# Padding v to pairs of chunks: one outer product and one near product where there were two

## What is computed

```python
state = 0
for t in range(S):
    cur = u * k[t] outer v[t]
    y[t] = r[t] @ (state + cur)
    state = w[t][:, None] * state + k[t] outer v[t]
x = y, heads side by side: (B*S, H*D)
x = moe(x)                       # 8 experts, 4 slots each
out = relu(x @ w_in) ** 2 @ w_out
```

## Time and profile before

| what | value |
|---|---|
| median of three runs | 556.15 us (553.27 to 556.74) |
| the profiled execution | 555.19 us, of it 553.4 us from the first to the last instruction |
| PE, busy | 485.5 us (88%) |
| ACT, busy | 332.8 us (60%) |
| DVE, busy | 334.6 us (60%) |
| the recurrence | to about 264 us; the rest is the two layers behind it |

### The profile page before, as it was taken

One profiled execution on the slowest core, in us unless ns is written; L12 is line 12 of the kernel. 1 busy time (PEld: TensorE's weight loads), 2 busy tenths in 40 slices (PEclk: granted clock), 3 DMA queues, 4 the chain that ended last, 5 costly groups with the idle time before them and its releaser, 6 DMA issues.

```text
span 553.4 us, 18757 instructions
## 1 busy us (share of the span) xinstructions
PE 485.5 (88%) x7850; PEld 425.1 (77%) x7850; DVE 334.6 (60%) x583; ACT 332.8 (60%) x689; POOL 13.7 (2%) x21
## 2 busy tenths in 40 slices
PE   1778889798989898678698879999999999999996
PEld 0557768677777777667333469999999999999996
DVE  5688868587878788925341167555555555555552
ACT  1787677686868687434221276656565656565653
POOL 9000000000000000000000000000000000000000
PEclk9998989798989899959889979999999999999999
DMA  6885565736262621293799730101010101010101
GB/s 112 146 213 103 150 113 152 137 70 117 57 118 52 114 56 34 59 403 136 238 390 369 260 114 1 44 1 44 1 43 2 43 0 43 0 43 1 44 1 43
DMA packets 119788, 56.23 MB, mean 102 GB/s; under 512 B 102944, under 2 KB 116256, under 8 KB 119328
## 3 DMA queue, kind: packets, MB, share of 16 engines
q1 hardware_dynamic: 116512, 42.54, 31.1%
q10 hardware_dynamic: 3200, 12.58, 6.1%
HBM read 50.38 MB, written 4.72 MB: 100 GB/s over the span
## 4 chain that ended last, share of the span: by engine, by line
PE 72%; ACT 11%; issue 7%; SPq 4%; DVE 4%; DMA 0%; ACTq 0%; DVEq 0%
PE bank L707 12%; PE bank L708 12%; PE bank L709 12%; ACT wide L802 4%; PE ybank L485 4%; PE lbank L468 4%; PE ybank L501 4%; PE lbank L451 4%; PE bank L697 4%; SPq L289 4%; PE tbank L402 3%; PE tbank L415 2%; PE bank L646 2%; PE bank L623 2%; ACT wl L743 2%
## 5 line engine op out<-in xcount | busy, mean ns | idle before, releaser
L707 PE MATMUL bank<-wo_high,h_high 128*128 128x384 f32 x384 | 129.6, 337 | 1.8 <-DVE h_low L1207 1.6
L708 PE MATMUL bank<-wo_low,h_high 128*128 128x384 f32 x384 | 129.0, 336 | 0.0
L709 PE MATMUL bank<-wo_high,h_low 128*128 128x384 f32 x384 | 128.9, 336 | 0.0
L953 ACT ACTIVATE h_relu<-bank 128x384 f32<-128x384 f32 x128 | 62.9, 492 | 74.4 <-PE bank L697 74.1
L1205 DVE CAST h_high<-h_sq 128x384 fp32r<-128x384 f32 x128 | 46.0, 359 | 96.7 <-PE bank L709 88.0
L1041 DVE TENSOR_TENSOR rk<-rk,wl 112x768 f32<-112x768 f32 x80 | 76.3, 954 | 36.7 <-PE lbank L468 19.9
L707 PEld LDWEIGHTS bank<-wo_high,h_high 128*128 128x128 f32 x384 | 72.6, 189 | 3.2 <-issue 2.7
L1207 DVE TENSOR_TENSOR h_low<-h_sq,h_high 128x384 fp32r<-128x384 f32 x128 | 71.5, 558 | 4.5
L708 PEld LDWEIGHTS bank<-wo_low,h_high 128*128 128x128 f32 x384 | 72.7, 189 | 0.0
L709 PEld LDWEIGHTS bank<-wo_high,h_low 128*128 128x128 f32 x384 | 72.5, 189 | 0.0
L957 ACT ACTIVATE h_sq<-h_relu 128x384 f32<-128x384 f32 x128 | 67.4, 527 | 4.1
(11 more groups left out here) (123 smaller groups left out, 532.5 us busy)
## 6 DMA issues: line engine op xcount, KB each, us to landing
w_sb<-in_moe_w_dram ACTq DMA_DIRECT2D x8, 1536.0 KB, 8.7
w_hi<-in_moe_w_dram SPq DMA_DIRECT2D x16, 384.0 KB, 8.0
nat<-in_w_dram SPq DMA_DIRECT2D x64, 72.0 KB, 2.4
nat<-in_r_dram SPq DMA_DIRECT2D x64, 72.0 KB, 2.5
nat<-in_k_dram SPq DMA_DIRECT2D x64, 72.0 KB, 2.4
v_tok<-in_v_dram SPq DMA_DIRECT2D x32, 144.0 KB, 3.1
w_lo<-in_moe_w_dram SPq DMA_DIRECT2D x1, 4608.0 KB, 16.8
out_dram<-o_sb SPq DMA_DIRECT2D x8, 576.0 KB, 3.0
```

The lines of the kernel that those rows point to most:

```text
L707: nc.tensor.matmul(acc, hi, wo_high[:, fb, :], start=(fb == 0), stop=False)
L708: nc.tensor.matmul(acc, hi, wo_low[:, fb, :], start=False, stop=False)
L709: last = nc.tensor.matmul(acc, lo, wo_high[:, fb, :], start=False, stop=(fb == NF - 1))
L953: nc.scalar.activation(h_relu[fb % 2][:], h_bank[fb % 2][:, 0:GT * P], ACT.Relu).then_inc(relu_done, 1)
```

## The change

v is kept with a padding: `v_tok` has for each block and head 96 columns. Tokens of the first chunk (partitions 0 to 63) hold v in columns 0 to 47 and zeros behind it, tokens of the second chunk (64 to 127) zeros and then v in columns 48 to 95. So one product with K = 128 rows and 96 columns gives both chunks' results side by side.

- `k_times_v`: 12 products of 48 x 96 in place of 22 of 48 x 48. Chunk c stands at column 48 (c mod 6) of bank c // 6, and `kv_out` copies it from there.
- `y_near`: 12 products of 64 x 96 in place of 24 of 64 x 48. Head h is now in PSUM partitions 64h to 64h+63, and the two chunks of a block side by side.
- `y_far`: the same 24 products with the same operands, but to PSUM partitions of the head instead of the chunk. The rows and the columns of the array that a product uses are now both those of head h.
- `y_to_x`: four copies of 64 partitions, one for each head and chunk, in place of two of 128.
- `load_v`: two transfers of 64 partitions per head in place of one of 128. Those of the first round move behind the inputs of the second round, and wait for GpSimd's zeros.
- GpSimd fills three more tiles (`v_tok`), and sets `ones` after the recurrence instead of as its second instruction.

```diff
-        v_tok = [[sb(f"v_tok{s}{b}", [P, PER, 2, D], c=att) for b in range(1 + s)] for s in range(2)]
+        v_tok = [[sb(f"v_tok{s}{b}", [P, PER, 2, 2, D], c=att) for b in range(1 + s)] for s in range(2)]
...
             def load_v(rd, s, h):
-                sp.dma_start(v_tok[s][rd % (1 + s)][:, :, h, :], v_v[rd * 4 + 2 * s + h]).then_inc(v_loaded[s], 16)
+                for par in range(2):
+                    sp.dma_start(v_tok[s][rd % (1 + s)][C * par:C * par + C, :, h, par, :], v_v[rd * 4 + 2 * s + h, par])\
+                        .then_inc(v_loaded[s], 16)
...
-            for s in range(2):
-                for h in range(2):
-                    load_v(0, s, h)
             sp.dma_start(phi_sb[:], phi.rearrange("(q p) n -> p q n", p=P)).then_inc(phi_loaded, 16)
...
+            sp.wait_ge(rows_zero, 13)
+            for s in range(2):
+                for h in range(2):
+                    load_v(0, s, h)
             for h in range(2):
                 load_v(1, 1, h)
...
-            pool.memset(ones[:], 1.0).then_inc(pool_const, 1)
...
-            for n, tile in enumerate(rt + rk0 + rk1 + rk2 + wide):
+            for n, tile in enumerate(rt + rk0 + rk1 + rk2 + wide + [v_tok[0][0], v_tok[1][0], v_tok[1][1]]):
                 if n:
                     pool.wait_ge(rows_zero, n)
                 pool.memset(tile[96:P] if n < 8 else tile[:], 0.0).then_inc(rows_zero, 1)
+            after_attention(pool)
+            pool.wait_ge(rows_zero, 13)
+            pool.memset(ones[:], 1.0).then_inc(ones_set, 1)
...
-                for c in range(NC - 1):
-                    i, par = divmod(c, 2)
-                    rows = slice(C * par, C * par + C)
+                for i in range(PER):
                     for h, (a, b) in enumerate(HEADS):
-                        last = nc.tensor.matmul(ybank[a:b, 512 * par + i * D:512 * par + (i + 1) * D],
-                                                k_tok[s][rows, i, a:b], v_tok[s][rd % (1 + s)][rows, i, h, :], start=True, stop=True)
+                        at = 512 * (i // GT) + (i % GT) * PW
+                        last = nc.tensor.matmul(ybank[a:b, at:at + PW], k_tok[s][:, i, a:b],
+                                                v_tok[s][rd % (1 + s)][:, i, h].rearrange("p par d -> p (par d)"),
+                                                start=True, stop=True)
...
                 for i in range(PER):
                     for h in range(2):
-                        for par in range(2):
-                            rows = slice(C * par, C * par + C)
-                            at = 512 * h + i * D
-                            last = nc.tensor.matmul(ybank[rows, at:at + D], aa[rd % 2][s][rows, PER * h + i, :],
-                                                    v_tok[s][rd % (1 + s)][rows, i, h, :], start=(i == 0), stop=False,
-                                                    skip_group_check=True)
+                        at = 512 * (i // GT) + (i % GT) * PW
+                        last = nc.tensor.matmul(ybank[HB * h:HB * h + C, at:at + PW], aa[rd % 2][s][:, PER * h + i, :],
+                                                v_tok[s][rd % (1 + s)][:, i, h].rearrange("p par d -> p (par d)"),
+                                                start=(i % GT == 0), stop=False, skip_group_check=True)
...
                             c = 2 * i + par
-                            rows = slice(C * par, C * par + C)
-                            at = 512 * h + i * D
-                            last = nc.tensor.matmul(ybank[rows, at:at + D], rk[rd % 3][s][a:b, 0, C * c:C * c + C],
-                                                    kv[s][a:b, :, c], start=False, stop=(i == PER - 1),
+                            at = 512 * (i // GT) + (i % GT) * PW + par * D
+                            last = nc.tensor.matmul(ybank[HB * h:HB * h + C, at:at + D], rk[rd % 3][s][a:b, 0, C * c:C * c + C],
+                                                    kv[s][a:b, :, c], start=False, stop=(i % GT == GT - 1),
                                                     skip_group_check=True)
...
-                for par, n in enumerate((NC // 2, NC // 2 - 1)):
-                    src = ybank[0:112, 512 * par:512 * par + n * D].rearrange("p (i d) -> p d i", d=D)
-                    dst = kv[s][0:112, :, 1 + par:2 + par + 2 * (n - 1):2]
-                    nc.scalar.activation(dst, src, ACT.Copy).then_inc(kv_evac[s], 1)
+                for half, n in enumerate((NC // 2, NC // 2 - 1)):
+                    src = ybank[0:112, 512 * half:512 * half + n * D].rearrange("p (c d) -> p d c", d=D)
+                    at = 1 + half * NC // 2
+                    nc.scalar.activation(kv[s][0:112, :, at:at + n], src, ACT.Copy).then_inc(kv_evac[s], 1)
...
                 for h in range(2):
-                    src = ybank[:, 512 * h:512 * h + PER * D].rearrange("p (i n) -> p i n", n=D)
-                    at = s * PW + h * D
-                    nc.scalar.activation(X[:, :, rd, at:at + D], src, ACT.Copy).then_inc(y_evac[s], 1)
+                    for par in range(2):
+                        src = ybank[HB * h:HB * h + C].rearrange("p (half x) -> p half x", half=2)[:, :, 0:GT * PW]\
+                            .rearrange("p half (i n) -> p half i n", n=PW)[:, :, :, par * D:par * D + D]
+                        at = s * PW + h * D
+                        dst = X[C * par:C * par + C, :, rd, at:at + D].rearrange("p (half i) n -> p half i n", half=2)
+                        nc.scalar.activation(dst, src, ACT.Copy).then_inc(y_evac[s], 1)
```

More of the change, by code:

```diff
@@ L39, in fused_kernel @@
     r_v, k_v, w_v = (a.rearrange("b h (g p i) d -> (b h) p g i d", p=P, i=2) for a in (r, k, w))
-    v_v = v.rearrange("b h (i p) d -> (b h) p i d", p=P)
+    v_v = v.rearrange("b h (i par p) d -> (b h) par p i d", par=2, p=C)
     T_ORDER = ([(s, 2, half) for s in range(2) for half in range(2)]
@@ L92, in fused_kernel @@
         u_col = sb("u_col", [P, 2 * ROUNDS])
-        ones = sb("ones", [P, P])
         comb = sb("comb", [P, SL])
@@ L160, in fused_kernel @@
         spread = sb("spread", [P, 2, 4, SL], F32R)
+        ones = sb("ones", [P, P])
         mx, mrow, mb = small[:, 0:1], small[0:1, 8:40], small[:, 40:72]
@@ L180, in fused_kernel @@
         rows_zero = sem("rows_zero")
+        ones_set = sem("ones_set")
         u_turned = sem("u_turned")
@@ L249, in after_attention @@
             for s in range(2):
-                eng.wait_ge(y_evac[s], 2 * ROUNDS)
+                eng.wait_ge(y_evac[s], 4 * ROUNDS)
         def xt_view(n):
@@ L329, in _ @@
                 for s in range(2):
-                    sp.wait_ge(y_evac[s], 2 * ROUNDS)
+                    sp.wait_ge(y_evac[s], 4 * ROUNDS)
                 sp.dma_start(debug, X[:].rearrange("p a b c -> p (a b c)")).then_inc(stored[0], 16)
@@ L370, in _ @@
             pool.memset(u_nat[:, HB + D:P], 0.0).then_inc(pool_const, 1)
-            pool.wait_ge(pool_const, 2)
+            pool.wait_ge(pool_const, 1)
             pool.affine_select(out=ident[:], in_=ident[:], compare_op=ALU.not_equal, fill=1.0, base=0,
@@ L420, in k_times_v @@
                 pe.wait_ge(t_evac, t_out[t_use["k", rd, s, 1]])
-                pe.wait_ge(v_loaded[s], 32 * (rd + 1))
+                pe.wait_ge(v_loaded[s], 64 * (rd + 1))
                 if rd == 0:
@@ L424, in k_times_v @@
                 if s == 0 and rd > 0:
-                    pe.wait_ge(y_evac[1], 2 * rd)
+                    pe.wait_ge(y_evac[1], 4 * rd)
                 if s == 1:
                     pe.wait_ge(kv_evac[0], 2 * (rd + 1))
-                for c in range(NC - 1):
-                    i, par = divmod(c, 2)
-                    rows = slice(C * par, C * par + C)
+                for i in range(PER):
                     for h, (a, b) in enumerate(HEADS):
-                        last = nc.tensor.matmul(ybank[a:b, 512 * par + i * D:512 * par + (i + 1) * D],
-                                                k_tok[s][rows, i, a:b], v_tok[s][rd % (1 + s)][rows, i, h, :], start=True, stop=True)
+                        at = 512 * (i // GT) + (i % GT) * PW
+                        last = nc.tensor.matmul(ybank[a:b, at:at + PW], k_tok[s][:, i, a:b],
+                                                v_tok[s][rd % (1 + s)][:, i, h].rearrange("p par d -> p (par d)"),
+                                                start=True, stop=True)
                 last.then_inc(kv_mm[s], 1)
@@ L563, in _ @@
                 pe.wait_ge(top_out[s], 2 * ROUNDS)
-                pe.wait_ge(y_evac[s], 2 * (ROUNDS - 1))
+                pe.wait_ge(y_evac[s], 4 * (ROUNDS - 1))
             turn_x(0, 4)
@@ L595, in _ @@
             pe.wait_ge(m_row, 1)
+            pe.wait_ge(ones_set, 1)
             nc.tensor.matmul(bank[3][:, 0:SL], ones[0:1, :], mrow, start=True, stop=True).then_inc(m_mm, 1)
+            pe.wait_ge(ones_set, 1)
             pe.wait_ge(d_exp, 2)
@@ L1218, in _ @@
                         split(gg * 2 + par, fb)
```

(2 more changed lines are left out.)

2 lines of the change are left out of this document (1 added, 1 removed).

## The result

The changed kernel takes 587.75 us (median of four runs, 586.39 to 588.62), the kernel before 556.44 beside it: a ratio of 1.059, 95% interval 1.056 to 1.062. The sign is the one forecast, the size is not: +31.3 us where +7 was predicted, and far above the range. The profiled execution of the changed kernel took 587.93 us, with a span of 585.8.

A forecast was written before the change was run, and what follows sets the result against it. No engine is full; a chain mostly through PE, crossing to ACT, bounds each round. Seven rounds at +0.75 give +5.3, tail +1.7, start -0.2: +6.8 on 555.19, 562.0, as median 563 us; range 553 to 573.

The forecast's parts named there:

- (3): Far blocks, both on the chain: slower on two array quarters instead of four, +0.80 or +1.98 us a round.
- (a): Far block: with one reader left, the weight load's 59 ns remain; 1.65 us, +0.40 each; chance 0.35.
- (4): `y_to_x`: four copies, each next start 0.30 us later, take 1.31 us; +0.60 each, +1.20 a round.
- (7): SP's transfers of v: twice as many issues, hidden in a queue that waits longer for far; 0, once bound +1.
- rival (e): v or the third round's inputs come late at 48 to 53 us: 3 us more, 566 us; chance 0.07.
- (1): `k_times_v`: 1.13 us against 0.74, +0.39; with the neighbour's gain +0.27 for set 0, 0 for set 1.
- (2): Near blocks: 24 records, 1.14 us against 1.60, -0.46; set 0 -0.58, set 1 -0.34.
- (6): PE's unexplained "issue" waits, 15.9 us in these rounds: 0.6 us a round taken back, bounds 0 and 2.3.
- rival (c): PE's stalls go, a round gains 2.3 us: 551, down to 542 us; sign: waits under 5 us; chance 0.08.
- (8): The start: ACT's first copy comes 0.24 us earlier without `ones` ahead of GpSimd's eighth tile.
- (9): The tail: last outer products, near, far and last `y_to_x` add +1.7 us in all.
- Rival (b): Far block: 84 ns belong to each stream, half the quarters give half the pace; 2.24 us, 571 us; chance 0.30.

The follow-up runs named there:

- experiments 1 to 3: Far reading neighbouring elements: 577.77 us in the changed kernel, 553.64 in the kernel before; third, far writing its head's PSUM half, in the kernel before: 569.06 us.
- experiment 6: The changed kernel with two copies to X of 128 partitions through the new pattern instead of four of 64: 572.8 us, ratio 1.029.
- (4): The kernel before with its two copies to X of 128 partitions cut into four of 64: 575.55 us, ratio 1.034.
- experiment 5: The changed kernel with three of the last round's weight transfers issued behind the second `y_to_x`: 579.49 us, ratio 1.041.
- 8: The changed kernel with contiguous far reads, two copies of 128 partitions and the last round's weights issued later, all together: 553.92 us, ratio 0.994.
- 10: The same three edits together in the changed kernel as in 8, plus the outer product and its copies as before: 551.65 us, ratio 0.992.

## Why the prediction was wrong, step by step

**(3) Far: the wrong one of two readings, and the main failure of judgement.** The prediction wrote down both, 1.65 and 2.24 us, and took (a) because "the near block is the nearest row". The nearest row had the same quarters, K, weights and columns, but not the one thing that the block's own row said was peculiar, the operand with 48 bytes from element to element. Measured: 2.29 us. 84 ns per quarter with four at work, 86 with two, and 61 and 60 in the same two cases without the stride (experiments 1 to 3). So the block went from 1.25 to 2.29 us because half of the array was left and each stream kept its own pace. Alone, in the kernel before, that is worth 13.2 us. The Trainium skill (SBUF — State Buffer, the part on cachelines), which the prediction set against (a), says that an access in a new 16-byte line pays; this case agrees, with 84 and 86 ns beside 61 and 60.

**(4) `y_to_x`: right mechanism, term mis-sized by far.** +0.60 us each was taken from the distance of 0.30 us between copies of 128 partitions. It is 0.43 between copies of 64, so +0.99. The trace of before already had narrower rows that I didn't read for this: on ACT's timeline `widen`, 48 partitions, takes 1.07 us for two of 0.53 each, with no overlap. Off by 0.39 us 16 times, which makes 15.2 us of the 9.0 in the sum: experiment 6 has 15.0. In the kernel before the four copies cost 19.7 (4), and the 4 us more are not explained.

**(7) The transfers: an unseen resource.** "In a queue that waits longer than that for far: 0" holds in the first rounds and fails in the last. There it was not the issue that mattered but the DMA engines, where v's packets take turns with those of the weights, and a first transfer of half the size gets half as much through before the weights begin. The prediction looked at 48 to 53 us for a late transfer (rival (e)), and there nothing waits; the late one is at 274. 8.3 us (5).

**(1) The outer product.** Its length was right, 1.16 against 1.13 at the full clock. But in six rounds the group costs 7.0 us more and not 4.7 (12 times 0.39), because set 0's stands at the lower clock more often: 1.46, 1.43, 2.13 and 2.01 us, at granted clocks of 0.78, 0.81, 0.50 and 0.57, in rounds where all but one were 0.74 us long before. These stand behind waits for ACT of 1.1 to 1.6 and of 0.6 to 0.7 us; that the waits bring the clock down was not tried alone. With the long copies undone, 8 against 10 shows 2.3 us in all.

**(2) Near** was right in its length, 1.19 and 1.21 against 1.14, and -4.8 us in six rounds against the -5.5 of the sum. It wasn't tried alone.

**(6) The stalls.** Over the seven rounds that the prediction counted they fell from 15.9 to 3.6 us, the stop for v left out: 1.8 a round against the 0.6 that I took. By the prediction's own sign, under 5, that is rival (c), and yet the time went far in the other direction: a stall that goes is worth only as much as the next wait leaves of it. Why they go is not shown.

**(5), (8), (9).** `kv_out`'s pair is 0.72 us instead of 0.76, within the bounds. The start is not earlier but later at the first mark, +1.0 us, which no term had. The tail is +6.3 instead of +1.7: behind the stop of 8.15 us the two outer products take 2.16 us each instead of 1.20 and 0.74, 2.4 more; two far blocks 2.1, the copies 1.0, near -0.8, and 1.6 that I can't assign.

**The sum again with what was measured.** Rival (b) stood at 571, with far right and the rest as in the prediction. Add the stop for v, 8.3, and the copies, 15.0 to 19.7 in place of 9.0, and it comes to 585 to 590; measured 587.75. This is bookkeeping after the fact: the terms (1), (6), (8) and (9) were each off too, by 1 to 9 us, and cancel in part. The prediction named the far block's length as the sign to look at, and it did say (b) at once. Most of the rest that was wrong lay in places where I had written 0, or had taken a spacing from a row of another shape.

## What to carry to other kernels

When two readings of one row differ by more than the whole gain, the row that differs from its neighbours is the one to explain: pick the reading that accounts for its peculiarity, not the one from the neighbour that lacks it. Splitting an instruction by partitions multiplied its full time on ACT here, since neither its length nor its start was shared; look for narrower rows in the trace you have before you price it. Splitting a transfer lets less of it through before a large one of another queue begins. That must be looked up where the slack is smallest, which was here in the last round, behind the steady ones. Layouts that put a product's input half and output half under the same index halve the part of the array in use: list the (input half, output half) pairs of every block before and after.

## What the runs showed of the hardware

- An ACT instruction on few partitions holds up the next. Behind copies of 128 partitions the next copy to X starts 0.1 us before the end (0.307 us apart at 0.41 us each); behind 96, 64, 48 or 32 the next starts 0.02 us after it (0.43 apart for these copies), and nowhere in these traces earlier. The one ahead decides: an instruction of 128 partitions behind `widen` (48) also starts 0.02 us after its end, and one of 32 behind one of 112 starts 0.05 us before it. The overlap behind 112 or 128 is not always taken: the copy at 121.00 in the earlier trace rows starts 0.03 us after the pair ahead of it.
- A stride of 48 bytes in a matmul's moving operand of 48 f32 columns costs each stream, 84 to 86 ns for a record instead of 60 to 61, whether two or four quarters of the array are at work.
- Two queues that fill the DMA engines take turns by packets: 733 packets of 192 bytes went beside 734 of about 4 KB in 8 us. So a 72 KB transfer in small packets, issued amid three of 1.5 MB on another queue, landed after 17.0 us, where the same one without them took at most 3.2 (experiment 5).
